# Attention and two MLPs on one core: other places for the attention blocks, output steps, weight steps and additions of the first MLP

## What is computed

```python
# attention inside chunks of 64 positions, for each batch and head
scores = (q_c @ k_c.T) / sqrt(64); scores -= max(scores)
attn = exp(scores) / (sum(exp(scores)) + 1e-09)
x = attn @ v_c                          # becomes 2304 x 512
# first MLP
h = x @ w_in;  x = (h - tanh(h)) @ w_out
# second MLP
h = x @ w2_in; out = (h * tanh(softplus(h))) @ w2_out
```

## Time and profile before

| | before |
|---|---|
| median of 3 runs | 905.92 us (905.13 to 906.49) |
| the profiled execution | 898.54 us |
| its span, first to last instruction | 896.8 us |
| TensorE busy with matmuls | 821.9 us (92% of the span) |
| VectorE, ScalarE, GpSimd busy | 616.2, 376.6, 184.2 us |
| mean granted TensorE clock | 0.975 of full speed |

### The profile page before, as it was taken

One profiled execution on the slowest core, in us unless ns is written; L12 is line 12 of the kernel. 1 busy time (PEld: TensorE's weight loads), 2 busy tenths in 40 slices (PEclk: granted clock), 3 DMA queues, 4 the chain that ended last, 5 costly groups with the idle time before them and its releaser, 6 DMA issues. The chain is left out here.

```text
span 896.8 us, 13616 instructions
## 1 busy us (share of the span) xinstructions
PE 821.9 (92%) x5298; PEld 749.6 (84%) x5298; DVE 616.2 (69%) x871; ACT 376.6 (42%) x539; POOL 184.2 (21%) x227
## 2 busy tenths in 40 slices
PE   7999667867778889989999999999999999999998
PEld 7999666867777778979989979898888989888896
DVE  6776634637767665747666578888877777777775
ACT  4444322323333333424443355544645344453543
POOL 3331223321533324305533000212000000000000
PEclk9999988989999999989999999999999999999999
DMA  7553334651545535648888943548734239442401
GB/s 248 187 180 116 105 106 143 212 189 48 187 177 188 188 130 200 221 173 313 325 315 322 367 157 118 181 171 302 308 141 158 89 114 378 153 165 83 154 12 71
DMA packets 50816, 165.80 MB, mean 185 GB/s; under 512 B 8000, under 2 KB 11840, under 8 KB 50752
## 3 DMA queue, kind: packets, MB, share of 16 engines
q1 hardware_dynamic: 40896, 129.26, 39.0%
q0 software_dynamic: 9856, 35.66, 11.8%
HBM read 110.36 MB, written 50.59 MB: 179 GB/s over the span
## 5 line engine op out<-in xcount | busy, mean ns | idle before, releaser
L1535 PE MATMUL psum<-w_lo,w_hi 128*128 128x384 f32 x288 | 97.6, 339 | 0.0
L1536 PE MATMUL psum<-w_hi,w_lo 128*128 128x384 f32 x288 | 97.1, 337 | 0.0
L1534 PE MATMUL psum<-w_hi 128*128 128x384 f32 x288 | 96.4, 335 | 0.7 <-DVE pool_words L1190 0.7
L1419 PE MATMUL psum<-w_hi 128*128 128x384 f32 x192 | 67.1, 350 | 13.9 <-DVE pool_words L1065 4.1
L1555 PE MATMUL psum<-w_hi,g_lo 128*128 128x512 f32 x192 | 76.1, 396 | 0.0
L1554 PE MATMUL psum<-w_lo,g_hi 128*128 128x512 f32 x192 | 75.9, 395 | 0.0
L1553 PE MATMUL psum<-w_hi,g_hi 128*128 128x512 f32 x192 | 74.9, 390 | 0.5 <-DVE pool_words L1005 0.4
L1357 PE MATMUL psum<-g_hi,w_hi 128*128 128x384 f32 x128 | 46.6, 364 | 30.2 <-DMA pool_words<-pool_words 30.2
L845 ACT ACTIVATE pool_words<-pool_words 128x768 f32<-128x768 f32 x48 | 40.3, 839 | 77.2 <-DVE pool_words L1158 77.2
L1162 DVE SCALAR_TENSOR_TENSOR pool_words<-pool_words 128x768 f32<-128x768 f32 x48 | 51.7, 1078 | 21.9 <-ACT pool_words L845 21.9
L1420 PE MATMUL psum<-w_lo,w_hi 128*128 128x384 f32 x192 | 66.2, 345 | 0.0
(11 more groups left out here) (173 smaller groups left out, 2232.9 us busy)
## 6 DMA issues: line engine op xcount, KB each, us to landing
w_hi<-s_hi SPq DMA_DIRECT2D x32, 896.0 KB, 5.0
w_lo<-s_lo SPq DMA_DIRECT2D x32, 896.0 KB, 7.3
pool_words<-w POOLq DMA_DIRECT2D x32, 256.0 KB, 3.5
pool_words<-w_out POOLq DMA_DIRECT2D x32, 256.0 KB, 4.2
s_hi<-w_hi SPq DMA_DIRECT2D x8, 896.0 KB, 5.5
s_lo<-w_lo SPq DMA_DIRECT2D x8, 896.0 KB, 7.3
w_hi<-t_hi SPq DMA_DIRECT2D x18, 384.0 KB, 5.5
w_lo<-t_lo SPq DMA_DIRECT2D x18, 384.0 KB, 6.6
```

The source lines that it names most:

```text
L1419: pe.matmul(ps, a_hi, t_hi_words[:, k, :], start=first, stop=False, skip_group_check=i in (M5, M3))
L1534: pe.matmul(ps, a_hi, t_hi_words[:, k, :], start=first, stop=False, skip_group_check=i in (M5, M3))
L1535: pe.matmul(ps, a_hi, t_lo_words[:, k, :], start=False, stop=False, skip_group_check=i in (M5, M3))
L1536: mm = pe.matmul(ps, a_lo, t_hi_words[:, k, :], start=False, stop=end, skip_group_check=i in (M5, M3))
```

## The change

In group 1 the places of blocks 9, 10 and 11 go from f = 9, 12, 14 to f = 10, 13, 15. The output steps of group 1 are three F tiles behind up to f = 10, there is none at f = 11, and they are four behind from f = 12; y1 of F tiles 12, 13 and 14 come after the group, that of 15 in pair 0. In group 1 the wait for the ordered blocks and the scores' inputs stands behind the output step instead of ahead of it. `keep_x(11)`, the first two `x1` splits and `shift(12)`, `exps(12)` come after the loop, in another order. In the pairs, with a block behind them, one output step more lies ahead of the block, others move. The first direct step goes from beside place 1 to beside place 0 and the third from `w1` to place 3; token steps go to place 1. On VectorE u3 comes ahead of the steps beside place 1, `turn_blocks` comes after c21, c22 comes ahead of the steps beside places 2 and 3, and c12 comes ahead of `minus1`. `block_move` only gives a name to the addresses of the 8 DMAs.

```diff
--- before.py
+++ after.py
@@ -16,7 +16,6 @@
 KT = D_MODEL // P
 FT = D_FF // P
 LAG1 = 2
-LAST_LAG = 4
 G_RING = 4
 STAGE1 = 4
 SCALE = 1.0 / HEAD_DIM ** 0.5
@@ -26,6 +25,8 @@
 
 
 PLAIN = 2
+
+OUTPUT_BEHIND = {f: f - 3 if f < 11 else f - 4 for f in range(3, FT) if f != 11}
 SUPERS = GROUPS // 2
 PAIRS = FT // 2
 ALL_PAIRS = SUPERS * PAIRS
@@ -56,12 +57,12 @@
 BUSY = (4, 3, 4, 3, 8, 2, 3)
 
 
-BLOCK_AT = {(0, 6): 3, (0, 10): 4, (0, 14): 5, (1, 1): 6, (1, 4): 7, (1, 7): 8, (1, 9): 9, (1, 12): 10, (1, 14): 11}
+BLOCK_AT = {(0, 6): 3, (0, 10): 4, (0, 14): 5, (1, 1): 6, (1, 4): 7, (1, 7): 8, (1, 10): 9, (1, 13): 10, (1, 15): 11}
 BLOCK_BEHIND = {0: 12, 2: 13, 3: 14, 4: 15, 5: 16, 6: 17}
 
 STEPS_AFTER = {1: (0, 0, 0, 0, 1, 1, 2), PAIRS + 1: (2, 2, 0, 0, 1, 1, 2)}
 STEPS_BESIDE_PAIR = (1, 1, 1, 1, 1, 1, 2)
-STEPS_BESIDE_BLOCK = (1, 1, 0, 0, 1, 1, 1)
+STEPS_BESIDE_BLOCK = (1, 1, 1, 1, 0, 1, 1)
 
 X_AT = {t: ((2, 1, 2, 2, 0)[t // GROUP_TILES - 1], t % GROUP_TILES) for t in range(GROUP_TILES, TILES)}
 X_THIRDS = ((1, 2), (2, 0))
@@ -97,12 +98,10 @@
 place_steps([("group", f) for f, _ in _G1], [step for _, step in _G1])
 for _q in range(1, PAIRS - 1):
     _d = parts("direct", _q + 1)
-    if _q == 2:
-        place_steps([(_q, 0)], _T[0][3:4])
-    place_steps([(_q, 1)], _d[0:1])
-    if _q in (1, 3, 4):
-        place_steps([(_q, 2)], [_T[0][{1: 2, 3: 5, 4: 6}[_q]]])
-    place_steps([(_q, 3), (_q, "w1")], _d[1:3])
+    place_steps([(_q, 0)], _d[0:1])
+    if _q < 5:
+        place_steps([(_q, 1)], [_T[0][{1: 2, 2: 3, 3: 5, 4: 6}[_q]]])
+    place_steps([(_q, 2), (_q, 3)], _d[1:3])
     if _q == 2:
         place_steps([(_q, "w1")], _T[0][4:5])
 place_steps([(PAIRS, 3), (PAIRS + 1, 1), (PAIRS + 1, 2), (PAIRS + 1, 3)], parts("weights", 2)[0:2] + [_T[1][0], ("weights", 2, 2)])
@@ -268,6 +267,10 @@
 
             t, k = {M1: (0, 0), M5: (0, 0), M3: (1, 2), M7: (1, 0), M6: (1, 2), M2: (0, 2), M4: (0, 2)}[i]
             return y_block(s, t, k)
+
+        def block_move(c, q1, k1):
+            rows, to_rows = (slice(c * CHUNK + 32 * h, c * CHUNK + 32 * h + 32) for h in (q1, k1))
+            return ordered_words[to_rows, q1 * 256:(q1 + 1) * 256], turned_blocks[rows, k1, :, :].rearrange("p h q -> p (h q)")
 
         def x_block(w, t, k):
             return third[X_THIRDS[w][t]][:, k:k + HALF_K, :]
@@ -508,9 +511,8 @@
                 for c in range(2):
                     for q1 in range(2):
                         for k1 in range(2):
-                            rows, to_rows = (slice(c * CHUNK + 32 * h, c * CHUNK + 32 * h + 32) for h in (q1, k1))
-                            sp.dma_start(ordered_words[to_rows, q1 * 256:(q1 + 1) * 256],
-                                         turned_blocks[rows, k1, :, :].rearrange("p h q -> p (h q)")).then_inc(blocks_ordered, 16)
+                            to, at = block_move(c, q1, k1)
+                            sp.dma_start(to, at).then_inc(blocks_ordered, 16)
 
             def wait_for_stores(k):
                 for b in range(3):
@@ -641,7 +643,9 @@
 
             def keep_x(t):
 
-                if t < TILES - 1:
+                if t == 11:
+                    act.wait_ge(scores_ready, t + 2)
+                elif t < TILES - 1:
                     act.wait_ge(shifted, t + 2)
                 act.wait_ge(values_ready, t + 1)
 
@@ -746,9 +750,6 @@
                         keep_x(t)
                     if g == 0 and f == FT - 1:
                         split_x_hi()
-                    if g == 1 and f == FT - 1:
-                        x1_hi(0, 0)
-                        x1_hi(0, 1)
                     tanh(n)
                     if g == 0 and f < FT - 2:
                         split_chunk_hi(f + 2)
@@ -834,6 +835,10 @@
             tanh(0)
             for g in range(PLAIN):
                 mlp1_group(g)
+            keep_x(11)
+            x1_hi(0, 0)
+            x1_hi(0, 1)
+            exps(12)
             for place in (2, 3, 4):
                 x1_hi(0, place)
             for q in range(PAIRS1):
@@ -923,6 +928,8 @@
                 scores = attention_banks(t)[0].rearrange("p m (i k) -> p m i k", i=4)
                 if 0 < t < GROUP_TILES:
                     dve.wait_ge(shifted, t)
+                if t == 12:
+                    dve.wait_ge(x_next_done, 9)
                 dve.tensor_reduce(out=row_max[:, :, :], in_=scores, op=ALU.max, axis=AX.X).then_inc(max_done, 1)
                 dve.wait_ge(max_done, t + 1)
                 if t == GROUP_TILES:
@@ -1024,11 +1031,8 @@
                         shift(scores_of)
                     if g == 0 and f == FT - 1:
                         split_x_lo()
-                    if g == 1 and f == FT - 1:
-                        x1_lo(0, 0)
-                        x1_lo(0, 1)
                     minus_tanh(n)
-                    if scores_of is not None and scores_of < 12:
+                    if scores_of is not None:
                         normalise(scores_of)
                         turn_blocks(scores_of)
                     if g == 0 and f < FT - 2:
@@ -1112,19 +1116,19 @@
                     x1_lo(0, 6)
                 if scored < TILES:
                     normalise(scored)
+                take1_u3(q)
                 beside_pair_lo(q, 1)
-                take1_u3(q)
+                if q == PAIRS + 1:
+                    keep_wide_y(0)
+                take1_c21(q)
                 if scored < TILES:
                     turn_blocks(scored)
-                if q == PAIRS + 1:
-                    keep_wide_y(0)
+                take1_c22(q)
                 beside_pair_lo(q, 2)
-                take1_c21(q)
                 beside_pair_lo(q, 3)
-                take1_c22(q)
+                take1_c12(q)
+                minus1(2 * q)
                 beside_pair_lo(q, "w1")
-                minus1(2 * q)
-                take1_c12(q)
                 lo1(2 * q)
 
             shift(0)
@@ -1142,6 +1146,9 @@
             minus_tanh(0)
             for g in range(PLAIN):
                 mlp1_group(g)
+            x1_lo(0, 0)
+            x1_lo(0, 1)
+            shift(12)
             for place in (2, 3, 4):
                 x1_lo(0, place)
             normalise(12)
@@ -1360,22 +1367,26 @@
                 mm.then_inc(y_step, 1)
 
             def mlp1_group(g):
-                lag = LAST_LAG if g == PLAIN - 1 else LAG1
                 for f in range(1, FT):
                     hidden(g, f)
                     scores_only = g == 0 and f == FIRST_SCORES_AT
                     if scores_only:
                         wait_for_scores(GROUP_TILES)
-                    if (g, f) in BLOCK_AT:
+                    if g == 0 and (g, f) in BLOCK_AT:
                         wait_for_values(BLOCK_AT[g, f])
                         wait_for_scores(BLOCK_AT[g, f] + 1)
-                    if f >= lag:
-                        y1(g, f - lag)
-                    elif f < LAG1 and g > 0:
-                        y1(g - 1, FT + f - LAG1)
+                    if g == 0 and f >= LAG1:
+                        y1(g, f - LAG1)
+                    if g == 1 and f < LAG1:
+                        y1(0, FT + f - LAG1)
+                    if g == 1 and f in OUTPUT_BEHIND:
+                        y1(g, OUTPUT_BEHIND[f])
                     if scores_only:
                         scores(GROUP_TILES)
                     if (g, f) in BLOCK_AT:
+                        if g == 1:
+                            wait_for_values(BLOCK_AT[g, f])
+                            wait_for_scores(BLOCK_AT[g, f] + 1)
                         values(BLOCK_AT[g, f])
                         scores(BLOCK_AT[g, f] + 1)
                 if g == 0:
@@ -1451,12 +1462,10 @@
                 for place in range(7):
                     product1(q, place)
                     if q == 0 and place == 5:
-                        y1(PLAIN - 1, FT - 2)
+                        y1(PLAIN - 1, FT - 1)
                     for _ in range(after[place]):
                         if q > 0:
                             y1_wide(*steps.pop(0))
-                if q == 0:
-                    y1(PLAIN - 1, FT - 1)
                 if t is not None:
                     wait_for_values(t)
                     if t + 1 < TILES:
@@ -1499,8 +1508,8 @@
             hidden(0, 0)
             for g in range(PLAIN):
                 mlp1_group(g)
-            y1(PLAIN - 1, FT - 4)
-            y1(PLAIN - 1, FT - 3)
+            for f in range(FT - 4, FT - 1):
+                y1(PLAIN - 1, f)
             for q in range(PAIRS1):
                 mlp1_pair(q)
```

## The result

The changed kernel takes 898.78 us (median of 4, 897.82 to 901.48), the one before 905.52 us beside it; the ratio is 0.9932, 95% interval 0.9905 to 0.9959. It is faster, by 6.7 us where 31 were forecast.

A forecast was written before the change was run, and what follows sets the result against it. TensorE, busy 92% of the span, was taken as the bound, so time could come only from its gaps and slow-clock stretches. Gains 22 + 3 + 2 + 4 = 31 us off 905.9 gave 875 us, range 863 to 888.

The forecast's parts named there:

- Part 1: Plain group 1: longer cycles hold more work, block 12 starts at 195.3 instead of 217.5 us; gain 22 us.
- V6 to V9: Starts of the values of blocks 6 to 9 in group 1: 97.8, 114.4, 129.9 and 143.7 us.
- V10: Start of block 10's values in group 1: 158.9 us, 14.4 us cycle plus 0.8 for steps ahead of its shift.
- V11: Start of block 11's values in group 1: 173.6 us, a 14.7 us cycle with about 5 us of wait.
- V12: Start of block 12's values, behind group 1: 195.3 us, 21.7 us after block 11's.
- Part 2: Pairs 1 and 2: waits at places 5 and 6 go, u2's grows by 0.9 us; gain 3, bounds 0 and 6.
- Part 3: Block pairs 3 to 6: waits move to the block, pair 3 gains 3 to 4 us; gain 2, bounds -6 and +6.
- Part 4: Pairs 7 to 15: pair 9's wait for c22 and its slow window go; gain 4 us, bounds 1 and 5.5.
- The first rival: Group 1 and pairs: beside more GpSimd DMAs each ordering takes block 7's 9.4 us; 891 us, chance 0.17.
- The waits did not all go: Rival for all parts: the ordering lands within the longer cycle everywhere, gain 52 us, total 854 us; chance 0.08.
- the third, the port pair: Block pairs: GpSimd's additions hold VectorE ahead of the transpose, 3.0 us in each of four, 887 us; chance 0.10.
- The slower rival: Six pairs: first direct step, waiting for the raw weights' load, blocks u2 on VectorE; at 7 us each 918 us; chance 0.03.

The follow-up runs named there:

- experiment 6: Changed kernel with normalising and transposing directly behind minus1 in the pairs, plus group 1's three weights steps at f = 11, 12, 13: 877.19 us, ratio 0.9675 to the kernel before.
- experiment 3: Kernel before with only the pairs changed, plain group 1 as before: 912.65 us, ratio 1.0060 to the kernel before.
- experiment 7: Changed kernel, but TensorE makes 14 small products while waiting for the ordered block in pairs 3 to 6: 896.93 us, ratio 0.9888 to the kernel before.
- experiment 8: Changed kernel, but in pairs 3 to 6 GpSimd's raw-weights load waits until the ordered block has landed: 892.72 us, ratio 0.9876 to the kernel before.
- experiments 4, 11: Changed kernel with, in the pairs, normalise and turn_blocks directly behind minus1: 880.77 us; and with only turn_blocks moved, directly behind normalise: 889.48 us.
- Experiment 9: Changed kernel with VectorE's old order in pairs 7 to 15: 895.43 us, ratio 0.9889 to the kernel before.

## Why the prediction was wrong

The direction, the place of the gain and the wait that would take its place were right. Steps of parts 1, 3 and 4 failed: what a wait brings with it was sized too small, or counted nowhere, and parts 3 and 4 came out with the wrong sign.

**Part 1, group 1 (22 forecast, 12 by the two first profiles, 16 against the second profile of before).** V6 to V9 hold to 1.5 us: 98.2, 115.8, 131.1, 144.9. The step that failed is V10: "the steps at f = 9 and 10 now lie directly ahead of the block's shift on VectorE, 0.8 us by my count of their durations". Their durations are not what they cost. The step at f = 10 waits for its buffer's store, and the shift starts 3.4 us after the scores (149.47 against 146.09). It also moved the ordering into GpSimd's stores and load: 9.25 us from issue to landing, against the 7.0 us (162.59 to 169.62 in the trace before) that the 14.4 us of the forecast hold. Together they make a cycle of 20.1 us for 15.2 forecast; experiment 6 shows both go with the step. V11 is 1.3 us longer than counted, as the hidden step that the transpose waits for runs at the lower clock. V12 is 24.3 us behind V11 instead of 21.7; a further slow stretch falls on its products.

**Part 2 (3 forecast, 1.3 measured).** The wait for u2 in pair 1 grew to 4.0 us as counted (3.19 + 0.9), and a slow stretch around it, the named bound, took the rest: the stage's clock is 0.90 instead of 0.95. In the pair part alone (experiment 3) it is 0.95 again and the stage takes 33.1 us, 3.6 less than before, with the same wait of 4.0 us. So the sum of this part was right for an unchanged clock.

**Part 3 (gain 2 forecast, loss 8.2).** The mechanism stood in the text: the waits inside the pair move before L1312, since the transpose follows c21. The sizes: the terms of the forecast give a period of 21.0 us (19.3 + 1.2 + 0.5; its last paragraph has 20.5), and the last three have 23.6 to 24.2. The block itself takes 2.0 us instead of 1.2 and the transpose ends 14.2 instead of 13.1 us after the scores; both are the lower clock after the wait, which was counted nowhere in this part (in experiment 7, without it, they are 1.2 and 13.2 again). The ordering takes 7.3 to 7.8 us instead of 6.8, from GpSimd's load, expected in kind and sized too small (experiment 8). Pair 3 was to gain 3 to 4 us and gained 0.6 (24.8 us against 25.4): no `lo1` there takes long any more, but its block waits 4.82 us like the others. What should have raised suspicion: in a stage where a chain through TensorE, VectorE and the DMAs closes on itself, a wait before the block comes back in part through place 4. The larger miss is one of sight: VectorE's idle time behind `minus1` meant that the transpose could be anywhere, and that the block pairs of both kernels were bound by its place (experiments 4, 11).

**Part 4 (gain 4 forecast, loss 4 to 5 on TensorE).** The wait of pair 9 for c22 did go. The other pairs lost more than it gave; "elsewhere nothing waits" was read from the trace of before and is no statement about the trace of after, in a stage where the DMAs were three quarters busy. Experiment 9 gives 3 us of it to the order. What makes up the rest stays open.

**The rivals.** The first (the ordering stretches, 891 us) was nearest: it happened at block 10 and by 1 us in each block pair, but is not the whole. The first rival's own sum comes to 892 us (905.9 - 15 + 6 - 5), 1 us beside the 891 it states. The waits did not all go. Of the third, the port pair, there is a trace of the size of 0.2 us a pair: here VectorE's normalising multiplication beside an addition of GpSimd takes 0.92 us, where the same operation takes 0.69 us without one.

```profile
277.91 0.92 DVE L959 TENSOR_TENSOR pool_words<-pool_words,row_inv 128x512 f32<-128x512 f32 x1
```

```profile
277.54 0.74 POOL L395 TENSOR_TENSOR pool_words<-pool_words 128x256 f32<-128x256 f32 x1
```

The rule of the Trainium skill, "SBUF — State Buffer", section "SBUF: two separate sides", that of a VectorE operation with two SBUF inputs and a GpSimd operation the one that starts first has the shared ports and the other waits, agrees with these rows in kind: the addition began first, and VectorE's operation is 0.23 us longer, though the addition still ran for 0.37. At this size it decides nothing. The row of 3.98 us that this rival rested on the earlier trace rows began 1.3 us before the addition of the earlier trace rows, when an undisturbed 0.96 us would have been over, so the addition alone does not explain it, and " agree" says more than these rows show. It comes again in the second profile of the kernel before (3.97 us) and not in the changed kernel; what held it is not shown. The slower rival (u2 behind the first direct step) showed in pair 1 alone.

**The baseline.** The sum was set against one profiled execution, 7 us below the median of its runs. The second profile shows that the difference lay mostly in slow time of group 1, the very waits that the change was to take away, so part 1 was worth some 4 us more against the runs than against the profile.

## What to carry to other kernels

When a chain crosses several engines and closes on itself, look first for the earliest place at which each link could stand on its engine's list, above all where that engine is idle: here two lines moved by some 8 us of time gained 18 to 20 us, as much as all that was rebalanced in group 1 (1.9%, 17 us). A step is to be costed by when its inputs and its buffer are free, not by its duration, and everything behind it on the engine counts. A long wait of TensorE cost itself here and the slower work behind it, and where later work of the chain depended on that, it cost it again.

## What was not expected of the hardware

Ordering 8 pieces of 32 KB takes 6.2 us from the first issue to the last landing when no load of another queue is issued beside it (block 11 of the changed kernel; in experiment 8 with two token stores beside it), 7.3 to 7.8 us beside a load of 0.5 MB in the changed kernel (up to 8.3 in experiment 3), and 9.0 to 9.7 us beside stores and a load of together over 1 MB. In experiment 6 the late one is block 11's, issued at 166.27 us behind SyncE's own store of 1.8 MB. The same program's profiles differed by 5 us (896.8 and 901.8 us span) with the waits in the same places and another share of slow time (granted clock 0.975 and 0.967). Whether kernels with fewer waits scatter less is not shown: the four with the transpose first have spreads of 1.7 to 4.5 us in four runs each, the changed kernel 3.7 in four.
